# Gates' first loads moved to ScalarE, three slots for y, the first visit one block later, and a weights' piece split between slabs of x

## The reference, cut to what matters

```python
f = 1.0 / (1.0 + np.exp(-f_logit))
for t in range(S):
    state = f[:, :, t, :, None] * state + np.einsum('bhd,bhe->bhde', k[:, :, t], v[:, :, t])
    y[:, :, t] = np.einsum('bhd,bhde->bhe', q[:, :, t], state)
x = y.transpose(0, 2, 1, 3).reshape(B * S, H * D)       # 3072 tokens x 384
x = (1 / (1 + np.exp(-(x @ w_gate))) * (x @ w_val)) @ w_out      # 384 -> 1536 -> 384
h = x @ w_in
return (h * (1 / (1 + np.exp(-1.702 * h)))) @ w_out2             # 384 -> 2048 -> 384
```

## Time and profile before

| | |
|---|---|
| median of 3 runs | 978.14 us (978.11 to 3597.63) |
| the profiled execution | 977.86 us |
| its span, first to last instruction | 976.1 us |
| busy: TensorE / VectorE / ScalarE / GpSimd | 950.8 / 492.0 / 303.6 / 106.2 us |
| mean granted TensorE clock | 0.989 |

### The profile page before, as it was taken

One profiled execution on the slowest core, in us unless ns is written; L12 is line 12 of the kernel. 1 busy time (PEld: TensorE's weight loads), 2 busy tenths in 40 slices (PEclk: granted clock), 3 DMA queues, 4 the chain that ended last, 5 costly groups with the idle time before them and its releaser, 6 DMA issues.

```text
span 976.1 us, 17704 instructions
## 1 busy us (share of the span) xinstructions
PE 950.8 (97%) x7149; PEld 789.5 (81%) x7149; DVE 492.0 (50%) x876; ACT 303.6 (31%) x621; POOL 106.2 (11%) x125
## 2 busy tenths in 40 slices
PE   7799999999999999999999999999999999999997
PEld 4688998888888888888788888888888888888885
DVE  6787877556654755565332234344343443443433
ACT  3443332223222322322223343223232232232221
POOL 3211211111110111011003440000000000000000
PEclk8799999999999999999999999999999999999999
DMA  5552322210211211121022330010010100100000
GB/s 154 160 167 60 98 73 67 58 46 26 83 49 50 69 55 42 46 75 30 9 86 81 101 104 23 1 65 1 1 65 0 36 30 1 65 1 1 33 1 35
DMA packets 44005, 52.33 MB, mean 54 GB/s; under 512 B 8464, under 2 KB 33808, under 8 KB 43920
## 3 DMA queue, kind: packets, MB, share of 16 engines
q1 hardware_dynamic: 42192, 44.07, 15.5%
q10 hardware_dynamic: 1728, 7.08, 2.5%
HBM read 36.96 MB, written 9.44 MB: 48 GB/s over the span
## 4 chain that ended last, share of the span: by engine, by line
PE 90%; DVE 4%; issue 2%; ACT 1%; DMA 0%; SPq 0%; DVEq 0%; ACTq 0%
PE up_ps L958 16%; PE up_ps L960 16%; PE up_ps L959 16%; PE out_ps L958 12%; PE out_ps L960 11%; PE out_ps L959 11%; PE att_ps L951 3%; PE att_ps L918 2%; PE att_ps L940 1%; DVE w_lo L758 1%; PE turn_ps L897 1%; PE att_ps L930 1%; DVE prod L704 1%; DVE state L734 1%; ACT act_hi L622 1%
## 5 line engine op out<-in xcount | busy, mean ns | idle before, releaser
L958 PE MATMUL up_ps<-x_hi,w_hi 128*128 128x512 f32 (+1 forms) x792 | 295.0, 372 | 4.6 <-DVE act_f L806 2.2
L960 PE MATMUL up_ps<-x_hi,w_lo 128*128 128x512 f32 (+1 forms) x792 | 293.4, 370 | 0.0
L959 PE MATMUL up_ps<-x_lo,w_hi 128*128 128x512 f32 (+1 forms) x792 | 293.3, 370 | 0.0
L958 PE MATMUL out_ps<-act_hi,w_hi 128*128 128x512 f32 (+1 forms) x540 | 207.8, 385 | 0.7 <-DVE act_lo L813 0.7
L960 PE MATMUL out_ps<-act_hi,w_lo 128*128 128x512 f32 (+1 forms) x540 | 202.9, 376 | 0.0
L959 PE MATMUL out_ps<-act_lo,w_hi 128*128 128x512 f32 (+1 forms) x540 | 202.6, 375 | 0.0
L622 ACT CAST act_hi<-act_f 128x512 fp32r<-128x512 f32 (+1 forms) x180 | 106.6, 592 | 259.7 <-DVE act_f L806 187.3
L813 DVE TENSOR_TENSOR act_lo<-act_f,act_hi 128x512 fp32r<-128x512 f32 (+1 forms) x180 | 118.5, 658 | 118.5 <-ACT act_hi L622 118.5
L958 PEld LDWEIGHTS up_ps<-x_hi,w_hi 128*128 128x128 f32 x792 | 149.5, 189 | 32.7 <-DVE act_f L806 3.2
L960 PEld LDWEIGHTS up_ps<-x_hi,w_lo 128*128 128x128 f32 x792 | 149.7, 189 | 25.5
L959 PEld LDWEIGHTS up_ps<-x_lo,w_hi 128*128 128x128 f32 x792 | 149.8, 189 | 25.2
(11 more groups left out here) (68 smaller groups left out, 511.4 us busy)
## 6 DMA issues: line engine op xcount, KB each, us to landing
stage<-w SPq DMA_DIRECT2D x16, 384.0 KB, 3.3
stage<-w ACTq DMA_DIRECT2D x9, 576.0 KB, 4.2
f_raw<-f_t SPq DMA_DIRECT2D x96, 48.0 KB, 1.9
q_raw<-q_t SPq DMA_DIRECT2D x96, 48.0 KB, 1.9
k_raw<-k_t SPq DMA_DIRECT2D x96, 48.0 KB, 1.9
v_raw<-v_n SPq DMA_DIRECT2D x48, 96.0 KB, 2.2
x_raw<-x_dram SPq DMA_DIRECT2D x6, 768.0 KB, 4.8
out_t<-final SPq DMA_DIRECT2D x18, 256.0 KB, 2.2
```

The costliest lines, as they stand in the source:

```text
L958: pe.matmul(dst, w_hi[:, at:at + P], m_hi, start=first, stop=False)
L959: pe.matmul(dst, w_hi[:, at:at + P], m_lo, start=False, stop=False)
L960: return pe.matmul(dst, w_lo[:, at:at + P], m_hi, start=False, stop=last)
```

## The change

Five edits, all in the work up to the second block of group 0.

1. **f by ScalarE.** The loads of `f_raw` for units 0 to 7 leave the SP queue; a new `first_load_f(n)` issues them from ScalarE, between its `forget`s. VectorE clears `q_raw` and `k_raw` before `gate` and `floor`, so SP starts behind three clears instead of five.
2. **Weights' loads later.** `load_w1(0)` goes from behind `forget(2)` to behind `forget(3)`; `load_w1(1)` from behind `forget(3)` to behind `take_y(0)`; `load_w1(2)` from behind `forget(5)` to behind `take_y(3)`, with `load_w1(3)` behind the `w1_first_part(1)` that follows it.
3. **Three slots of `y_t`** (`YS = 3`), one semaphore each.
4. **First visit one block later.** Visit 8 stands in block 1 instead of 0, and with it its `take_k` and `forget(8)`; `prepare(6)` goes from ahead of the loop into block 0. From block 2 on all is as before.
5. **Piece 1 between slabs.** `w1_second_part(1)` stands between slab 0 and slabs 1 and 2 of x on VectorE, instead of behind all three.

```diff
@@ tables @@
-        for j in (0, 2, 4, 6, 8) if g == 0 else (0, 1, 3, 4, 5, 7, 8, 9):
+        for j in (1, 2, 4, 6, 8) if g == 0 else (0, 1, 3, 4, 5, 7, 8, 9):
...
-            forgets, prepares = {j: n + 3 for n, j in enumerate((0, 2, 4, 6, 8))}, {j: n + 2 for n, j in enumerate((1, 3, 5, 7, 9))}
+            forgets = {j: n + 3 for n, j in enumerate((1, 2, 4, 6, 8))}
+            prepares = {j: n + 1 for n, j in enumerate((0, 1, 3, 5, 7, 9))}
...
+        YS = 3
...
-        y_t = sb("y_t", [P, 2, W])
+        y_t = sb("y_t", [P, YS, W])
@@ SP @@
-                sp.wait_ge(gaps_set, 1)
-                load_f(0)
-                load_f(1)
-                sp.wait_ge(gaps_set, 5)
+                sp.wait_ge(gaps_set, 3)
                 load_kq(0)
-                load_f(2)
                 load_kq(1)
                 load_v(0)
-                load_f(3)
+                load_v(1)
                 load_kq(2)
-                load_v(1)
+                load_v(2)
                 load_kq(3)
-                load_v(2)
-                load_f(4)
+                load_v(3)
                 load_kq(4)
-                load_v(3)
-                load_f(5)
-                load_f(6)
                 move_y(0)
                 load_v(4)
+                move_y(1)
                 load_kq(5)
-                move_y(1)
                 load_v(5)
-                load_f(7)
                 move_y(2)
@@ ScalarE @@
+                def first_load_f(n):
+                    u = Unit(n)
+                    wait(act, gate_done, n - 1)
+                    for i in range(PAIR):
+                        act.dma_start(f_raw[rows[i], u.s, :], f_t[u.pair, i, :, u.tokens]).then_inc(f_loaded[u.s], 16)
...
-                    wait(act, y_moved[u.s], 16 * moves(u.s, n))
-                    act.copy(y_t[:, u.s, :].rearrange("p (c r t) -> p c r t", c=BLOCKS, r=SIDES),
+                    wait(act, y_moved[n % YS], 16 * moves(n % YS, n))
+                    act.copy(y_t[:, n % YS, :].rearrange("p (c r t) -> p c r t", c=BLOCKS, r=SIDES),
...
+                act.wait_ge(gaps_set, 1)
+                first_load_f(0)
 
                 act.wait_ge(warm_set, 1)
                 act.activation(y_t[:, 0, 0:1], x_raw[:, 0, 0:1], ACT.Sigmoid)
+                first_load_f(1)
                 forget(0)
+                first_load_f(2)
                 forget(1)
+                first_load_f(3)
                 take_k(0)
                 forget(2)
-                load_w1(0)
+                first_load_f(4)
                 take_k(1)
                 forget(3)
+                load_w1(0)
+                take_k(2)
+                first_load_f(5)
+                w1_first_part(0)
+                forget(4)
+                first_load_f(6)
+                take_y(0)
                 load_w1(1)
-                w1_first_part(0)
-                take_k(2)
-                forget(4)
-                take_y(0)
                 take_k(3)
                 forget(5)
-                load_w1(2)
+                first_load_f(7)
                 take_y(1)
                 take_y(2)
                 take_y(3)
+                load_w1(2)
+                w1_first_part(1)
                 load_w1(3)
-                w1_first_part(1)
                 take_k(4)
                 x_first_part(0)
@@ VectorE @@
-                x_second_part(0)
+                x_second_part(0, [0])
                 w1_second_part(1)
+                x_second_part(0, [1, 2])
                 prepare(5)
                 after_visit(7)
-                prepare(6)
```

More of the change, by code:

```diff
@@ L160, in gla_moe_moe2 @@
         y_taken = sem("y_taken")
-        y_moved = sems("y_moved", 2)
+        y_moved = sems("y_moved", YS)
         w1_loaded = sems("w1_loaded", 4)
@@ L226, in moves @@
         def moves(s, n):
-            return sum(MOVES[m % UG] for m in range(s, n, 2))
+            return sum(MOVES[m % UG] for m in range(s, n, YS))
         class Unit:
@@ L335, in load_f @@
                         u = Unit(n)
-                        wait(sp, gate_done, n - 1)
+                        sp.wait_ge(gate_done, n - 1)
                         for i in range(PAIR):
@@ L364, in move_y @@
                             sp.dma_start(x_raw[row:row + m, slab, u.in_group],
-                                         y_t[64 * i + at:64 * i + at + m, u.s, :]).then_inc(y_moved[u.s], 16)
+                                         y_t[64 * i + at:64 * i + at + m, n % YS, :]).then_inc(y_moved[n % YS], 16)
                 def store(group):
@@ L545, in forget @@
                     if n < 2:
-                        act.wait_ge(gaps_set, 3)
+                        act.wait_ge(gaps_set, 5)
                     wait(act, scan_done, n - 1)
@@ L574, in x_first_part @@
                             after = steps_of(group)[-1] * UG + min(k + 2, UG)
-                            for s in range(2):
+                            for s in range(YS):
                                 act.wait_ge(y_moved[s], 16 * moves(s, after))
                         act.copy(x_hi[:, group % 2, k, 0:n], x_raw[:, k, 0:n]).then_inc(x_hi_done, 1)
+                act.wait_ge(gaps_set, 1)
+                first_load_f(0)
                 act.wait_ge(warm_set, 1)
                 act.activation(y_t[:, 0, 0:1], x_raw[:, 0, 0:1], ACT.Sigmoid)
+                first_load_f(1)
                 forget(0)
+                first_load_f(2)
                 forget(1)
+                first_load_f(3)
                 take_k(0)
                 forget(2)
-                load_w1(0)
+                first_load_f(4)
                 take_k(1)
                 forget(3)
+                load_w1(0)
[5 more added lines that the diff above has]
+                take_y(0)
                 load_w1(1)
-                w1_first_part(0)
-                take_k(2)
-                forget(4)
-                take_y(0)
                 take_k(3)
                 forget(5)
-                load_w1(2)
+                first_load_f(7)
                 take_y(1)
@@ L689, in _ @@
                 dve.memset(f_raw[:, :, :], 30.0).then_inc(gaps_set, 1)
+                dve.memset(q_raw[:, :, :], 0.0).then_inc(gaps_set, 1)
+                dve.memset(k_raw[:, :, :], 0.0).then_inc(gaps_set, 1)
                 dve.memset(gate[:, :, :], 0.0).then_inc(gaps_set, 1)
                 dve.memset(floor[:, :, :], SAFE_PRODUCT).then_inc(gaps_set, 1)
-                dve.memset(q_raw[:, :, :], 0.0).then_inc(gaps_set, 1)
-                dve.memset(k_raw[:, :, :], 0.0).then_inc(gaps_set, 1)
                 for ps in (att_ps, out_ps):
@@ L745, in after_visit, with x_second_part @@
                         new_states(kept, v)
-                def x_second_part(group):
+                def x_second_part(group, slabs=range(KC)):
                     n = GROUPS1[group][1] if group < NG1 else N
-                    for k in range(KC):
+                    for k in slabs:
                         dve.wait_ge(x_hi_done, group * KC + k + 1)
```

## The result

| | before | changed |
|---|---|---|
| median | 978.12 us (10 runs) | 975.11 us (10 runs, 974.47 to 976.62) |
| profiled execution | 977.86 us | 974.81 us |
| its span | 976.1 us | 973.1 us |
| ratio, 95% interval | | 0.9974 [0.9964, 0.9984] |

What follows compares the result with a forecast made beforehand. VectorE's pace was taken to bound group 0, started when x is whole, with TensorE filling the rest. X −1.7 and VectorE's work −1.27 gave −3.0 us: median 975.2 us, likeliest 974.0 to 976.0, range 973.4 to 978.0.

Steps and rivals of the forecast that it cites:

- What leads in group 0: Group 0 goes at VectorE's pace, started when x is whole; TensorE fills the rest, which does not change.
- X: End of the last `x_lo` on VectorE: 35.52 us before, forecast 33.8, bounds 32.9 and 35.2.
- G: End of TensorE's last wait for VectorE in group 0: 88.80 us before, forecast near 85.8.
- Early loads: Ahead of group 0's visits: visit 2 starts at 13.5 for 15.95, visit 3 is 2.4 us earlier.
- The third slot: ScalarE takes y of unit 3 at 26.0 for 29.76, its 2.33 us wait gone; alone leaves SP late.
- SP and the moves: Unit 3's second move issued at 29.7, 2.7 us before, landing in 3.2 us beside the weights: X 1.7 us earlier.
- Piece 1's low part: On VectorE, hidden in the 2.09 us wait before slab 1, so 1.27 us leave the work after X.
- Visit and prepare: `prepare(6)` moves into block 0: price 0, first product about 2.9 us sooner, TensorE's 2.51 us wait vanishes.
- A: Unit 3's moves land late, in 4.6 us: X 35.2, gain 1.6 us, time 976.6; chance 0.27 together with D.
- B: Weights' piece 0 lands late, visits 3 to 6 gain nothing: slower, 979.0 to 980.6 us; chance 0.10.
- C: TensorE's granted clock stays full, visits 3 to 6 come 1.5 to 2 us shorter: 973.4 us; chance 0.18.
- D: Only the split pays: gain at X eaten whole, 1.27 us remain, 976.9 us; chance 0.27 together with A.

Runs made afterwards that it cites:

- pieces apart: Changed kernel with weights' piece 2 loaded behind forget(5) again, about 6 us ahead of piece 3: median 974.77 us, ratio 0.9972.
- pieces early: Changed kernel with weights' pieces 0 and 1 loaded behind forget(2) and forget(3) again, f still on ScalarE: median 974.66 us, ratio 0.9971.
- moves first: Changed kernel with SP's moves of y of units 2 and 3 ahead of unit 5 and 6 loads: median 974.78 us, ratio 0.9973.
- fewer keep-warm matmuls: Kernel with all three edits, but three instead of six keep-warm matmuls behind visit 6: median 973.15 us, ratio 0.9955.
- all three edits: Changed kernel plus SP's unit 2 and 3 moves first, weights' pieces 2 and 3 apart, piece 1's low part ahead of slab 0: 973.72 us, again 973.04.

## Why the prediction was right, and where its working was not

**What leads in group 0.** Right, and the firmest point: in every kernel in which X moved, G moved with it, and X to G stayed at 51.54 to 51.55 in the changed kernel and in four experiments that left VectorE's list and the clock alone (two slots, pieces apart, pieces early, moves first), over 1.9 us of X. It is not without exception. In four executions VectorE waited once for value matmuls at half clock, 0.26 to 0.48 us, and the stretch was 0.35 to 0.60 longer (f on SP, fewer keep-warm matmuls, the first run with all three edits and the one with the weights early as well). TensorE's 2.51 us wait at 40.09 was worth nothing, as the visit put back shows.

**Early loads.** Forecast visit 2 at 13.5 and visit 3 at 18.25; measured 13.70 and 18.39. The cause was half right: I gave it to SP's freed time and to the later weights together. With f on SP and the later weights, visits 2 and 3 began at 16.03 and 19.98; with f on ScalarE and the weights early, at 13.40 and 17.68 (before: 15.95 and 20.75). All of the gain at visit 2 is SP's time, which gets q and k of unit 2 out ahead of the weights; at visit 3 the later weights took back 0.7 of what SP's time gave.

**The third slot** was forecast to be no good without SP. With two slots and SP's new order ScalarE did not wait for one either: the third is worth nothing here.

**SP and the moves.** The step that failed in size: "SP comes 2.7 before, landing 3.2, X −1.7". Of the 1.06 us that X was late, 0.47 are the later issue (30.17 for 29.7, with one k issue that held the queue for 1.20), 0.61 the landing (3.81 for 3.2). My own range for the landing, 2.2 to 4.6, held it, and five executions gave 3.09 to 3.81: the value was low by 0.35 on average, the mechanism right. On the issue my sum took the f load's 2.07 us as its price and 2.1 for q and k. But 1.60 of the 2.07 were one slow issue, of a kind that came back in the new order, at a load of k or q of unit 5: 1.09 to 1.62 us in the changed kernel and in the six variants that keep these loads there, with f on SP too. Taking out a load that stood at the slow place did not take out the slow place.

**Piece 1's low part** 1.27: right, 1.28 and 1.29 in two runs. It kept 0.23 us of cover in one of them.

**Visit and prepare: "its price is 0".** Wrong by 0.45, in the kernel's favour. I took `prepare(6)` as a block of work that is the same wherever it stands. Its scan had taken 1.14 where that of `prepare(5)` took 0.68, and I did not ask why. It met GpSimd's `k_dec(5)`; a block later it does not.

**The sum.** Forecast −1.7 − 1.27 = −3.0. Measured at G: −0.66 − 1.27 − 0.45 = −2.4, and 0.6 in the rest that I cannot give to the change. That the total came out so near is luck.

**The rivals.** A (X 35.2, gain 1.6) was nearer to the profile at X, where 0.66 was gained, than my forecast. B's mechanism is real (piece 0 late by 1.3 to 1.5, visit 3 by 1.0 to 1.4), but not at the size that turns the sign. C: the clock was no better in the visits:

```profile
16.60:30.10 13.50, 10.36 (x165) 8.72 (x166) 6.64 (x20) 4.50 (x12) 5.05 (x6) 0.50 0.55 158
...
37.10:43.80 6.70, 6.33 (x76) 5.70 (x75) 5.72 (x12) 2.69 (x7) 2.20 (x3) 1.00 0.51 151
```

0.50 from 16.6 to 30.1, as in the earlier trace rows, so visits 3 to 6 took their old 7.7 us. From 37.1 to 43.8 it was 1.00 for 0.52, in a stretch that VectorE leads, and bought nothing: 1.28 and 0.45 us of the other edits fill the stretch's 1.74. The prediction's "a second fall in group 0 would cost little" fits the 0.35 to 0.60 us of the four executions above. D was its split alone: 1.29.

## What to carry to other kernels

Before summing edits, find the one moment that starts the longest run of a leading engine, and price each edit as a shift of that moment or as work taken from behind it. A small transfer on the way to it should not be issued shortly behind two large loads, even if these are issued from another engine: its landing went from 2.0 us to between 3.1 and 4.7 here. Taking the queue's own loads out of its way, or the large ones apart, each brought X 1.3 to 1.9 us forward in one profiled execution. Together, with the low part moved and the first weights early again, they took the ratio from 0.9974 to 0.9948. If one instance of an operation takes longer than its siblings (1.14 for 0.68), ask what stood beside it before calling a move free.

## What the runs showed of the hardware that I had not expected

- A 48 KB move inside SBUF, issued 3.5 to 3.7 us behind the second of two 576 KB loads, landed in 3.09 to 3.81 us (five executions); with the first of them 6.9 us earlier, in 1.95; issued 1.0 us behind the pair, in 4.72.
- A scan of 256 columns that starts while GpSimd works on two inputs from SBUF takes 1.14 us for 0.68. The same shift stands in the weights' low part of the kernels with all three edits: it started 0.2 us after a 0.72 us `k_dec` of GpSimd had started, and took 1.73 to 1.74 us for 1.35.
- One DMA issue on SP, of a load of unit 5, held its queue for 1.09 to 1.62 us in the changed kernel and six variants, with 0.42 to 0.58 for its neighbours; in the kernel before it was a load of f (1.60 us at 27.24). No wait in the traces explains it, and the cause stays open.
- The landing of the first of the 576 KB loads (piece 0, issued between 10.9 and 11.9) was 3.9 to 4.9 us in the changed kernel and seven of its variants, and 5.4 and 5.6 in the two executions of the kernel with all three edits.
